# Attention and two gated layers on one core: six units of 384 tokens in place of eight of 288

## The chip, the cores and the metric

The kernel runs on one core of one Trainium2 chip. The metric is the device time of one execution in microseconds, from all inputs in HBM to the last output row in HBM. Lower is better.

## What is computed

Three parts follow one another. The inputs are 4 sequences of 576 tokens, 8 heads of 64.

```python
def _attn_ref(q, k, v, w1, b1, w2):            # 4 x 8 x 576 x 64
    scores = scale * np.matmul(q, k.transpose(0, 1, 3, 2))
    rel = (pos[:, None] - pos[None, :]).astype(np.float32)
    x = (np.log1p(np.abs(rel)) / np.log1p(np.maximum(pos[:, None], 1.0)))[..., None]
    bias = np.maximum(x @ w1 + b1, 0.0) @ w2    # one 576 x 576 table for each head
    scores = scores + bias.transpose(2, 0, 1)[None]
    attn = np.exp(scores - np.max(scores, axis=-1, keepdims=True))
    attn = attn / (np.sum(attn, axis=-1, keepdims=True) + 1e-09)
    return np.matmul(attn, v)
def _moe_ref(x, w_in, w_out):                   # 2304 x 512, inner 2048
    h = x @ w_in
    return (h - np.tanh(h)) @ w_out
def _moe2_ref(x, w_gate, w_val, w_out):         # inner 1536
    g = x @ w_gate
    return (g * (1.0 / (1.0 + np.exp(-g))) * (x @ w_val)) @ w_out
```

## The kernel before, in words

All products are made from operands that are split in a high part (type fp32r) and a low part (the rest). A product of weights and activations is three matmuls (high by high, high by low, low by high). For the scores the high and the low part of q lie in the two halves of the partitions, so a score tile is two matmuls for each half of the keys.

**Stages.** (1) The bias tables are computed in 36 rounds and written to HBM (`bias_scratch`). (2) Attention alone for the first 8 heads. (3) The first layer of unit u beside the attention of unit u+1. (4) The first layer of the last unit alone, while the weights of the second layer are loaded and split. (5) The second layer on 6 blocks of 384 tokens; its result leaves from PSUM through ScalarE.

**Units.** A unit is 288 tokens, one half of a sequence. There are 8 (`UNITS`), with 8 heads each. The queries of a head are cut into three tiles of 96 rows (`QT`, `NQ`). The keys are 576 in five chunks of 128; the fifth starts at key 448, so its first 64 keys are there twice, and v has zeros for them.

**One tile of a head.** TensorE makes the scores (`scores`, L1077, 4 matmuls of 288 columns). VectorE adds the bias and takes the row maximum (`score`, L878). ScalarE takes the exponential and the row sum (`exp_tile`, L646). VectorE inverts the sum (`inverse`, L885 and L888). GpSimd multiplies the rows by it (`norm`, L546). TensorE transposes the tile in five pieces into PSUM (`transposed`, L1090). ScalarE copies the high part (`pt_high`, L654), and VectorE subtracts it for the low part (`pt_low`, L893). When the three tiles of a head are ready, TensorE multiplies them by v (`output`, L1100, ten matmuls of 288 columns, five for the high part and five for the low part); ScalarE copies one half of the result to other partitions (`o_part`, L670), and VectorE adds the other half (`x_out`, L906). GpSimd splits k (L529, L531) and v (L538, L540).

**One chunk of the first layer.** There are 16 chunks of 128 hidden values. `hidden_pieces` (L1124) is 4 pieces of 3 matmuls into `ps_h`; then `tanh` (ScalarE, L659), `gated` (VectorE, L899), `g_high` (ScalarE, L664), `split_g` (GpSimd, L551), and `model_pieces` (L1143), again 4 pieces of 3 matmuls, into `ps_y`.

**The order of the work** is written out by hand. A slot is one call of a function `slot` on each engine; every engine runs its own list in order. In stage 3 a slot holds the attention of one head and two chunks of the layer. On TensorE it is: transposes of tile 0 of the head before, scores of tile 0, 4 pieces; the same for tile 1, 4 pieces; for tile 2, 3 pieces; then `output`, then the pieces that are left. In stage 2 a slot has no pieces, and TensorE makes `output` of the head before the last ahead of the transposes. There `output` goes to `ps_y`, and tiles 0, 1 and 2 are transposed into three different banks; in stage 3 all three tiles and `output` share the bank `ps_pt`.

At the end of a unit VectorE copies `x_stage` to `x_hi` (`x_high`, L915) and subtracts for `x_lo` (`x_low`, L920). The result of a unit goes from `ps_y` through ScalarE (`y_out`, L676) to `y_stage` and by DMA to HBM (`store_y`). The 28 weight tiles of the first layer that are not split in stage 1 are split in the slots of the first unit, four to a slot: four copies on ScalarE (`w1_high`, L613), three subtractions on VectorE (`w1_low`, L839) and one on GpSimd (L556).

Units 1 to 5 of stage 3 and pairs of blocks of stage 5 are loops of the program (`Fori`, L329 and L341); the first unit, the last two and the last two blocks are written out. All DMAs are issued by SyncE in one order: for each head v, k, q, and three bias tiles (`load_head`, L402).

## Time and profile before

| | us |
|---|---|
| median of 3 runs | 1258.95 (1256.47 to 1260.03) |
| the profiled execution | 1256.5 |
| its span, first to last instruction | 1254.4 |
| TensorE busy | 1194.2 (95%) |
| VectorE, ScalarE, GpSimd busy | 637.9, 595.3, 573.3 |
| granted TensorE clock, mean | 0.992 |

The profiled execution lies 2.1 us above its own span and 2.5 us below the median of the runs. "Busy" is the time in which at least one instruction of the engine ran; matmuls overlap, so the mean duration of one matmul is longer than its share of the busy time, and the pace is better read from the start of one group to the start of the next.

### The profile page before, as it was taken

To read this page: it belongs to the slowest core of one execution; us is meant where nothing else is said; L and a number is where in the kernel's file an instruction comes from. 1 tells how busy PE (TensorE), PEld (TensorE's weight loads), DVE (VectorE), ACT (ScalarE), POOL (GpSimd) and SP (SyncE) were. 2 spreads that over 40 slices of the span, in tenths; PEclk is the share of its full clock that TensorE was granted. 3 is DMA by queue.
4 is the path that set the end of the run, shared out by engine and by line. 5 is a ranking of instruction groups with operands and counts; after the bars stand their busy time and mean duration, and the time that the engine had idled before them with its cause. 6 is when DMAs were issued, how large, how long until landed. Compare 5 with 4: busy or idle time off the path is not lost.

```text
span 1254.4 us, 25061 instructions
## 1 busy us (share of the span) xinstructions
PE 1194.2 (95%) x8400; PEld 1127.0 (90%) x8400; DVE 637.9 (51%) x1575; ACT 595.3 (47%) x1301; POOL 573.3 (46%) x664
## 2 busy tenths in 40 slices
PE   5767799999999999999999999999999999999999
PEld 2346699999999999999999999999999999999998
DVE  8967888666666666666666644521211212112111
ACT  6966687655655656555656545521212222122212
POOL 2047699666666766776666644211111111111111
PEclk9989899999999999999999999999999999999999
DMA  5888354444444443444444434300100000000000
GB/s 165 242 257 244 107 182 122 129 123 123 141 122 122 140 120 109 135 120 128 121 119 137 123 125 152 120 26 1 40 11 25 25 25 25 0 26 1 26 1 26
DMA packets 69153, 125.01 MB, mean 100 GB/s; under 512 B 8544, under 2 KB 32096, under 8 KB 69088
## 3 DMA queue, kind: packets, MB, share of 16 engines
q1 hardware_dynamic: 69088, 124.16, 33.4%
q8 instruction: 39, 0.64, 0.2%
q14 instruction: 26, 0.21, 0.1%
HBM read 104.07 MB, written 20.05 MB: 99 GB/s over the span
## 4 chain that ended last, share of the span: by engine, by line
PE 84%; DVE 5%; issue 3%; POOL 3%; ACT 3%; DMA 1%; SPq 1%; POOLq 0%; DVEq 0%
PE ps_h L1124 14%; PE ps_y L1143 14%; PE ps_s L1215 12%; PE ps_y L1226 12%; PE ps_s L1077 7%; PE ps_h L1215 6%; PE ps_pt L1215 6%; PE ps_pt L1090 6%; PE ps_pt L1100 5%; DVE feat L847 3%; POOL fr L551 1%; POOL prob L546 1%; DVE prob L878 1%; ACT wbuf L654 1%; DVE wbuf L893 1%
## 5 line engine op out<-in xcount | busy, mean ns | idle before, releaser
L588 POOL TENSOR_TENSOR fr<-x_stage,fr 128x384 fp32r<-128x384 f32 x72 | 72.9, 1012 | 380.1 <-ACT fr L777 380.1
L546 POOL TENSOR_SCALAR prob<-prob,rowinv 96x576 f32<-96x576 f32 x192 | 149.6, 784 | 197.6 <-DVE rowinv L888 196.9
L1143 PE MATMUL ps_y<-fr,wbuf 128*128 128x288 f32 x1536 | 225.4, 295 | 1.1 <-POOL fr L551 0.4
L1124 PE MATMUL ps_h<-fr,wbuf 128*128 128x288 f32 x1440 | 219.9, 296 | 0.7 <-DVE fr L920 0.7
L1143 PEld LDWEIGHTS ps_y<-fr,wbuf 128*128 128x128 f32 x1536 | 210.4, 188 | 2.9 <-POOL fr L551 2.8
L1124 PEld LDWEIGHTS ps_h<-fr,wbuf 128*128 128x128 f32 x1440 | 201.1, 189 | 1.7 <-issue 1.0
L893 DVE TENSOR_TENSOR wbuf<-ps_pt,wbuf 128x480 fp32r<-128x480 f32 x176 | 115.6, 657 | 151.2 <-ACT wbuf L654 150.6
L654 ACT ACTIVATE wbuf<-ps_pt 128x480 fp32r<-128x480 f32 x176 | 100.5, 571 | 185.2 <-PE ps_pt L1090 185.0
L1226 PE MATMUL ps_y<-wbuf,fr 128*128 128x512 f32 x648 | 162.1, 395 | 0.0
L646 ACT ACTIVATE prob<-prob,negmax 96x576 f32<-96x576 f32 x192 | 147.8, 770 | 10.2 <-DVE negmax L878 10.1
L551 POOL TENSOR_TENSOR fr<-g_b,fr 128x288 fp32r<-128x288 f32 x128 | 112.2, 876 | 79.2 <-ACT fr L664 79.1
L1226 PEld LDWEIGHTS ps_y<-wbuf,fr 128*128 128x128 f32 x648 | 120.8, 188 | 22.8
L878 DVE CUSTOM_DVE_ANT_0 prob<-ps_s,biasb 96x576 f32<-96x576 f32 x179 | 133.2, 744 | 2.8 <-PE ps_s L1077 2.2
L1077 PE MATMUL ps_s<-wbuf,fr 128*96 128x288 f32 x672 | 126.2, 310 | 2.5 <-DVE negmax L878 2.5
L1023 DVE TENSOR_TENSOR x_stage<-ps_h,x_stage 128x384 f32<-128x384 f32 x36 | 20.1, 557 | 180.8 <-ACT x_stage L774 180.8
L1090 PE MATMUL ps_pt<-ident,prob 96*128 96x96 f32 x880 | 102.9, 247 | 7.4 <-POOL prob L546 5.4
L1023 DVE TENSOR_TENSOR x_stage<-ps_s,x_stage 128x384 f32<-128x384 f32 x36 | 20.1, 557 | 160.8 <-ACT x_stage L774 160.8
L1090 PEld LDWEIGHTS ps_pt<-ident,prob 96*128 96x128 f32 x880 | 90.8, 141 | 11.0 <-POOL prob L546 6.7
L1077 PEld LDWEIGHTS ps_s<-wbuf,fr 128*96 128x96 f32 x672 | 86.4, 164 | 4.3 <-DVE negmax L878 4.3
L531 POOL TENSOR_TENSOR wbuf<-k_raw,wbuf 128x576 fp32r<-128x576 f32 x59 | 86.8, 1471 | 4.9
L774 ACT ACTIVATE x_stage<-ps_h 128x384 f32<-128x384 f32 x36 | 17.7, 491 | 141.7 <-PE ps_pt L1215 141.7
L1100 PE MATMUL ps_pt<-wbuf,fr 128*128 128x288 f32 x560 | 83.2, 295 | 0.0
(111 smaller groups left out, 1832.0 us busy)
## 6 DMA issues: line engine op xcount, KB each, us to landing
biasb<-bias_scratch SPq DMA_DIRECT2D x192, 216.0 KB, 3.9
k_raw<-k_t SPq DMA_DIRECT2D x59, 288.0 KB, 2.8
bias_scratch<-w_raw SPq DMA_DIRECT2D x72, 144.0 KB, 2.8
v_raw<-v_p SPq DMA_DIRECT2D x64, 160.0 KB, 3.4
q_raw<-q_t SPq DMA_DIRECT2D x59, 144.0 KB, 2.6
w_raw<-w_chunks SPq DMA_DIRECT2D x16, 512.0 KB, 6.1
prob<-w_chunks SPq DMA_DIRECT2D x8, 768.0 KB, 4.2
y_scratch<-y_stage SPq DMA_DIRECT2D x8, 576.0 KB, 4.5
```

Source lines behind the costliest of these rows:

```text
L546: eng.tensor_scalar(prob[0:QT, par, t, :], prob[0:QT, par, t, :], rowinv[0:QT, par, t:t + 1], 1.0, ALU.mult, ALU.mult).then_inc(p_norm, 1)
L551: eng.tensor_tensor(g_lo[i], g_b[:, i, :], g_hi[i].bitcast(F32), ALU.subtract).then_inc(p_glo, 1)
L646: eng.activation(prob[0:QT, par, t, :], prob[0:QT, par, t, :], ACT.Exp, scale=-1.0, bias=negmax[0:QT, par, t:t + 1], accum_out=rowsum[0:QT ...
L878: eng.tensor_tensor_reduce(out=pairs(prob[0:QT, par, t, :]), in0=score_bank(par, t, moe)[0:QT, :, 0:T1], in1=pairs(biasb[0:QT, par, t, :]) ...
L893: eng.tensor_tensor(pt_lo[:, :, cols], by_chunk(bank), pt_hi[:, :, cols].bitcast(F32), ALU.subtract)\
L1077: mm = eng.matmul(bank[0:QT, a, 0:T1], q[:, t * QT:(t + 1) * QT], k[:, a * T1:(a + 1) * T1], start=i == 0, stop=i == 1)
L1090: mm = eng.transpose(bank[:, c * QT:(c + 1) * QT], prob[0:QT, par, t, KEY0[c]:KEY0[c] + P], ident[0:QT, 0:QT])
L1100: mm = eng.matmul(bank[:, 0:T1], vv[:, c, :, :].rearrange("p a d -> p (a d)"), pt[:, c, :], start=i == 0 and c == 0, stop=i == 1 and c == ...
L1124: mm = eng.matmul(hidden_bank(u, c)[:, 0:T1], w[:, cols], x[:, d, :], start=d == 0 and i == 0, stop=d == KC - 1 and i == 2)
L1143: mm = eng.matmul(ps_y[:, d, 0:T1], w[:, cols], g[c % 2], start=c == 0 and i == 0, stop=c == C1 - 1 and i == 2)
L1215: mm = eng.matmul(bank, w[:, cols], y[:, d, :], start=d == 0 and i == 0, stop=d == KC - 1 and i == 2)
L1226: mm = eng.matmul(ps_y[:, t, :], a[c % 2][:, t * P:(t + 1) * P], w, start=c == 0 and i == 0, stop=c == C2 - 1 and i == 2)
```

## The change

**Units.** There are six units of 384 tokens (`TOK`, `PARTS`). Units 0 to 3 are the first 384 tokens of each sequence: 8 heads each, of three tiles of 128 rows. Units 4 and 5 are the last 192 tokens of two sequences: 16 heads each, of two tiles of 96 rows. Heads stay 64 in all; tiles are 160 (were 192). In stage 3 a slot of units 0, 1 and 2 holds a head of 384 tokens and two chunks of the layer; a slot of units 3 and 4 holds a head of 192 tokens and one chunk.

**Keys.** A tile of 128 rows is transposed in four pieces of 128 keys. The last 64 keys of its three tiles are transposed together behind the third tile (`transposed_end`, three transposes into `ps_pt`); ScalarE copies the high part into one half of the partitions of `pt_end`, VectorE puts the low part into the other half, v has its last 64 keys in both halves, and one matmul serves for both parts. `output` of such a head is nine matmuls of 384 columns; of a head of 192 tokens it is ten of 192.

**Order.** In stage 3 ScalarE now does `exp_tile` and `tanh` ahead of the next tile's `pt_high`, and VectorE `inverse` and `gated` ahead of the next `pt_low`. `x_high` goes to ScalarE for three of its four chunks.

**Storage.** `prob` is a ring of 6 tiles, `biasb` a ring of 4. `x_stage` and `y_stage` are one buffer: `y_out` of unit u-1 waits for `x_low` of unit u, and the first `o_part` of unit u+1, in the same slot, waits for the store of y, which is now two or more DMAs (its first chunk by itself). `o_part` writes into `x_stage` itself. A bias tile of 128 rows is two DMAs, q of a long head two, v three.

**Loads.** Eight of the 16 weight chunks of the first layer are loaded in stage 1 (were six), the others from head 9 on. The first four bias tiles are loaded behind round 27 (were three).

**Loops.** The loops over units and blocks are written out.

```diff
-UNITS = 2 * B
-HEADS = UNITS * H
+TOK = 384
+PARTS = B * S // TOK
+def list_heads():
+    heads, tiles = [], 0
+    for u in range(PARTS):
+        pieces = [(u, 0, TOK // P, P)] if u < B else [(2 * (u - B) + i, TOK, (S - TOK) // QT, QT) for i in range(2)]
+        for h in range(H):
+            for i, (seq, row0, nt, rows) in enumerate(pieces):
+                heads.append(Head(len(heads), u, h, seq, row0, i * nt * rows, nt, rows, tiles))
+                tiles += nt
+    return heads, tiles
...
         def slots(slot, edge):
+            for u in range(PARTS):
+                attended = HEADS[FIRST_OF[u + 1]:FIRST_OF[u + 2]] if u + 1 < PARTS else [None] * H
+                per = C1 // len(attended)
+                for j, v in enumerate(attended):
+                    after = HEADS[v.n + 1:v.n + 3] if v is not None else []
+                    q, p = (after + [None, None])[:2]
+                    slot(q, v, p, [(u, j * per + i) for i in range(per)])
...
+            def transposed_end(hd, moe):
+                eng.wait_ge(v_pt, rounds(hd, hd.nt if moe else 1))
+                for t in range(hd.nt):
+                    mm = eng.transpose(ps_pt[:, tile_cols(hd, t)], prob[:, (hd.tile0 + t) % PR, S - P:S], ident[:, :])
+                mm.then_inc(e_pt, 1)
+            def output(hd, moe):
+                eng.wait_ge(v_pt, all_rounds(hd))
...
+                for part in range(2):
+                    for c in range(chunks_of(hd)):
+                        mm = eng.matmul(bank, vv[:, c, :, :]..., pt_of(hd, part)[:, c, :], ...)
+                if ended(hd):
+                    mm = eng.matmul(bank, vv[:, FULL, :, :]..., pt_end, start=False, stop=True)
```

The slot on TensorE:

```diff
+            def slot(q, v, p, moe):
+                pieces = []
...
+                gaps = ([4, 0, 2] if moe[0] == (0, 0) else [4, 4, 2]) if len(moe) == 2 else [4, 2]
+                for t, gap in enumerate(gaps):
+                    if v is not None and t < v.nt:
+                        transposed(v, t, moe)
+                    if q is not None and t < q.nt:
+                        scores(q, t, moe)
+                    layer_work(gap)
+                if v is not None:
+                    if ended(v):
+                        transposed_end(v, moe)
+                        layer_work(3)
+                    output(v, moe)
                 layer_work(len(pieces))
```

The slot on ScalarE in stage 3 (`when[i]` is the tile number behind which chunk i's tanh stands):

```diff
+                for t in range(end + 1):
+                    if t < v.nt:
+                        pt_high(v, t, moe)
+                    for k in (tiles[-1:], tiles[1:2], [])[t]:
+                        w1_high(k)
+                    if t == 1 and ends_unit:
+                        y_out(moe[0][0] - 1)
+                    for i, (u, c) in enumerate(moe):
+                        if when[i] == t - 1:
+                            g_high(u, c)
+                    if t == end:
+                        if p is not None:
+                            q_high(p, moe)
+                        if ended(v):
+                            pt_high_end(v)
+                        if one:
+                            o_part(v, moe)
+                    if q is not None and t < q.nt:
+                        exp_tile(q, t)
+                    for k in (tiles[0:1], tiles[2:3], [])[t]:
+                        w1_high(k)
+                    for i, (u, c) in enumerate(moe):
+                        if when[i] == t:
+                            tanh(u, c)
```

The slot on VectorE in stage 3, and the two waits that the shared buffer brings to ScalarE:

```diff
+                for t in range(end + 1):
+                    if t < v.nt:
+                        pt_low(v, t, moe)
+                    if q is not None and t < q.nt:
+                        score(q, t, moe)
...
+                    if t == end:
+                        if ended(v):
+                            pt_low_end(v)
+                        if p is not None:
+                            q_low(p, moe)
+                        if one:
+                            x_out(v, moe)
+                    if q is not None and t < q.nt:
+                        inverse(q, t)
+                    for k in (tiles[0:1], tiles[1:2], [])[t]:
+                        w1_low(k)
+                    for i, (u, c) in enumerate(moe):
+                        if when[i] == t:
+                            gated(u, c)
...
+            def o_part(hd, moe):
+                if hd.unit > 1:
+                    eng.wait_ge(d_y_first if hd.h < 2 else d_y_rest, Y_SUM[hd.unit - 1])
             def y_out(u):
+                eng.wait_ge(v_xlo, 2 * min(u + 2, PARTS))
```

## Rows read from the trace of the kernel before

**Rows 1.** The page's first part: busy time, share of the span, instructions

```profile
PE 1194.2 (95%) x8400; PEld 1127.0 (90%) x8400; DVE 637.9 (51%) x1575; ACT 595.3 (47%) x1301; POOL 573.3 (46%) x664
```

**Rows 2.** Busy time by stage: stretch, length, five engines (x), PEclk, DMA share, GB/s

```profile
0.00:76.00 76.00, 50.70 (x609) 25.49 (x609) 67.05 (x139) 62.38 (x91) 7.75 (x15) 1.00 0.72 214
76.00:143.60 67.60, 43.88 (x296) 38.24 (x294) 51.24 (x143) 38.36 (x90) 48.34 (x60) 0.87 0.75 219
143.60:740.00 596.40, 590.04 (x4720) 584.91 (x4720) 395.20 (x1095) 368.26 (x883) 422.21 (x502) 1.00 0.44 125
740.00:797.70 57.70, 55.93 (x406) 53.97 (x405) 26.76 (x33) 30.20 (x51) 22.11 (x17) 1.00 0.51 175
797.70:1254.40 456.70, 453.61 (x2377) 424.38 (x2375) 97.66 (x167) 96.10 (x190) 72.87 (x72) 1.00 0.06 21
```

**Rows 3.** Timeline of TensorE in one slot of stage 3: start, us, engine, line

```profile
429.05 1.49 PE L1100 MATMUL ps_pt<-wbuf,fr 128*128 128x288 f32 x10
...
430.77 1.74 PE L1143 MATMUL ps_y<-fr,wbuf 128*128 128x288 f32 x12
432.36 0.58 PE L1090 MATMUL ps_pt<-ident,prob 96*128 96x96 f32 x5
432.71 0.75 PE L1077 MATMUL ps_s<-wbuf,fr 128*96 128x288 f32 x4
433.30 1.75 PE L1124 MATMUL ps_h<-fr,wbuf 128*128 128x288 f32 x12
...
437.43 0.58 PE L1090 MATMUL ps_pt<-ident,prob 96*128 96x96 f32 x5
...
439.57 1.49 PE L1100 MATMUL ps_pt<-wbuf,fr 128*128 128x288 f32 x10
```

**Rows 4.** Chain that ended last, stage 5: start, us, what

```profile
810.40 2.11 PE ps_pt L1215 x12
812.51 2.10 PE ps_y L1226 x9
```

**Rows 5.** Timeline of ScalarE and VectorE, end of the same slot

```profile
438.05 0.57 ACT L654 ACTIVATE wbuf<-ps_pt 128x480 fp32r<-128x480 f32 x1 [0.93 <-PE ps_pt L1090]
...
438.65 0.66 DVE L893 TENSOR_TENSOR wbuf<-ps_pt,wbuf 128x480 fp32r<-128x480 f32 x1 [0.60 <-ACT wbuf L654]
```

**Rows 6.** Groups by line: xcount | busy us, mean ns of one | idle before

```profile
L613 ACT ACTIVATE wbuf<-w_raw 128x512 fp32r<-128x512 f32 x32 | 18.5, 622 | 0.0
L839 DVE TENSOR_TENSOR wbuf<-w_raw,wbuf 128x512 fp32r<-128x512 f32 x25 | 20.1, 804 | 0.0
```

**Rows 7.** Timeline of TensorE at the first slot of units 1 and 3

```profile
228.49 0.60 PE L1090 MATMUL ps_pt<-ident,prob 96*128 96x96 f32 x5 [0.92 <-POOL prob L546]
...
400.16 0.60 PE L1090 MATMUL ps_pt<-ident,prob 96*128 96x96 f32 x5 [0.92 <-POOL prob L546]
```

**Rows 8.** Timeline of VectorE and GpSimd in stage 4

```profile
784.39 1.75 DVE L928 TENSOR_TENSOR wbuf<-prob,wbuf 128x1536 fp32r<-128x1536 f32 x1
785.03 1.77 POOL L551 TENSOR_TENSOR fr<-g_b,fr 128x288 fp32r<-128x288 f32 x1 [2.75 <-ACT fr L664]
```

**Rows 9.** Groups of GpSimd by line

```profile
L546 POOL TENSOR_SCALAR prob<-prob,rowinv 96x576 f32<-96x576 f32 x192 | 149.6, 784 | 197.6 <-DVE rowinv L888 196.9
L551 POOL TENSOR_TENSOR fr<-g_b,fr 128x288 fp32r<-128x288 f32 x128 | 112.2, 876 | 79.2 <-ACT fr L664 79.1
```

**Rows 10.** Timeline of VectorE and TensorE in stage 2

```profile
79.84 0.75 DVE L878 CUSTOM_DVE_ANT_0 prob<-ps_y,biasb 96x576 f32<-96x576 f32 x1 [3.62 <-DMA biasb<-bias_scratch]
...
129.84 0.66 DVE L893 TENSOR_TENSOR wbuf<-ps_y,wbuf 128x480 fp32r<-128x480 f32 x1 [0.56 <-ACT wbuf L654]
130.56 1.58 PE L1100 MATMUL ps_y<-wbuf,fr 128*128 128x288 f32 x10 [1.29 <-DVE wbuf L893]
...
137.74 2.77 PE L1100 MATMUL ps_y<-wbuf,fr 128*128 128x288 f32 x10 [3.83 <-DVE wbuf L893]
```

**Rows 11.** Timeline of SyncE's queue in a slot of stage 3

```profile
433.96 1.36 SPq L399 DMA_DIRECT2D biasb<-bias_scratch  x3
```

More of the change, by code:

```diff
@@ L347, in attention_layers_kernel, with steps @@
+        def steps(step):
+            for v in range(V2):
+                step(v, v % 2, v == V2 - 1)
         SPLIT_AT = 4
@@ L581, in _ @@
             eng.sem_inc(p_alo, 1)
-            slots(eng, slot, None)
-            with eng.Fori(0, V2) as v:
+            slots(slot, None)
+            for v in range(V2):
                 for c in range(C2):
@@ L969, in slot @@
-                if qk:
-                    inverse(n, par, 0)
-                for k in tiles[1:2]:
-                    w1_low(k)
-                if pv:
-                    pt_low(n - 1, 2, banks[2])
-                if qk:
-                    score(n, par, 2, moe)
-                    inverse(n, par, 1)
-                if prep:
-                    q_low(n + 1, 1 - par, moe)
-                if pv and not last:
-                    x_out(n - 1, 1 - par, o_bank, x_chunk)
-                w2_lows(w2_splits[0])
@@ L986, in slot @@
+                if not one:
+                    x_out(v, moe)
                 for k in tiles[2:3]:
                     w1_low(k)
-                w2_lows(w2_splits[1])
-                if pv and last:
-                    x_high(moe[0] + 1, 0)
-                    x_out(n - 1, 1 - par, o_bank, x_chunk)
-                    x_low(moe[0] + 1, 0)
-                    x_high(moe[0] + 1, 1)
-                    x_low(moe[0] + 1, 1)
-                if qk and last:
-                    inverse(n, par, 2)
+                if late(moe):
+                    x_low(moe[0][0] + 1, 0)
@@ L1197, in _ @@
             eng.sem_inc(e_out, 2)
-            slots(eng, slot, edge)
-            for piece in model_pieces(UNITS - 1, C1 - 1):
+            slots(slot, edge)
+            for piece in model_pieces(PARTS - 1, C1 - 1):
                 piece()
```

1012 lines of the change are left out of this document (522 added, 490 removed).

## The prediction

> **What bounds the kernel now.** I read the page's busy line first: TensorE is busy for 95% of the span, no other engine for more than 51% [rows 1]. By stage [rows 2]: bias tables 76 us, attention alone 67.6, layer beside attention 596.4, the last unit alone 57.7, second layer 456.7. TensorE is busy for 99% of the third and the last, but for only 65% of the second, where its clock also drops (mean 0.87). So three fifths of the time is a question of TensorE's instructions, and stage 2 is one of waits between engines.
>
> The pace is read from starts. One slot of stage 3 takes 10.52 us from `output` to `output`, without a wait [rows 3]. In it five transposes take 0.36 (0.072 each), four scores 0.585, and twelve layer matmuls of 288 columns 1.60 (0.133 each). `output` takes 1.33 (ten at the same 0.133). In stage 5 twelve matmuls of 384 columns take 2.11 (0.1758 each) and nine of 512 take 2.10 (0.2335) [rows 4]. A line through the three is 6 to 7 ns per matmul plus 0.44 ns per column: the cost follows the columns, and little is fixed. The skill page "TensorE: Matmul & The Clock Gate" (Back-to-back issue gap) gives N/2.4 + 2.5 ns, so a smaller fixed part; by it the removal of 768 matmuls would bring 2 us where my line brings 5. My sum uses the rows.
>
> **TensorE's work from slot 9 to the second layer.** Before: 56 slots of 10.52 are 589.1, and 32 groups of 1.60 for the last unit 51.2; sum 640.3. The stretch is 654.1 (143.6 to 797.7 [rows 2]), and the transposes and scores of its first slot lie ahead of it, 1.9 at the low clock (twice 0.36 + 0.585). So some 15.7 us of 656.0 are stalls.
> After:
> - Layer: 6 units x 32 groups x 2.11 = 405.1 (was 409.6).
> - Long head: scores 3 x 0.585 = 1.76; fifteen transposes of 128 columns. Bounds for one are 0.072 (the row, if the load sets it) and 0.096 (in proportion to columns); I take 0.080, nearer to the row of the same 128-column load: 1.20. Nine matmuls of 384 are 1.58. Sum 4.54, for 24 heads 108.9 (bounds 106 to 115).
> - Short head: 2 x (0.36 + 0.585) and ten matmuls of 192 columns, between 0.072 and 0.133, 0.091 by the line: 2.80, for 32 heads 89.6 (84 to 103).
> Sum 603.6, which is 36.7 less. A long slot becomes 12.98, a short one 7.02.
>
> **Stalls of that stretch, after.**
> - Every slot: what `output` waits for. Now the last tile's transposes start at 437.43, its copy at 438.05, and the subtraction ends at 439.31, 1.88 later; `output` comes 2.14 behind the transposes [rows 3, 5]. That leaves 0.26. After, a short slot has 0.36 + 0.585 + six matmuls (1.055) = 2.00 there. The long slot has 2.04 ahead of the packed transposes, which reuse the bank, against about 1.97 (longer transposes and copies). The work queued ahead of the copy also changes: an exponential and tanh now come first. Walking both slots through, each on its own list, I find the copies just in time. I take 0.1 a slot, 5 us; bounds 0 and 0.6 a slot (34 us).
> - First unit: three weight copies of 0.62 on ScalarE and two subtractions of 0.80 on VectorE [rows 6] now stand between tile 0's exponential and tile 2's subtraction. My walk gives a stall of 1.2 a slot, for seven slots 8.4; bounds 0 and 1.9 a slot.
> - Unit ends: now a unit's first transposes wait 0.92 for `norm` [rows 7]. After, the shared x/y buffer puts `o_part` of the first head behind `y_out` and a store. In the long slots (13 us) this is hidden. In a short slot `ps_y` is complete about 3.1 in, the first copy waits for `x_low`, and its DMA lands some 3 us later. I take 3 us at each of two such ends, 0.6 at two long ones, 1.7 at the last: 9 (bounds 4 and 15).
> - Last unit: `split_g` takes 1.77 where VectorE runs a weight subtraction of 1.75 [rows 8] and 0.88 in the mean [rows 9]. With 2.11 a group the round trip of about 3.9 fits under two groups (4.22); before, about 3.45 stood against 3.2. So 1 us is left of it. Start of the stage, clock low: 3.
> Sum 26.4, 10.7 more than now.
>
> **Stage 2.** Tiles stay 27, since 128 rows cost the lanes what 96 do. A slot takes 7.18 (130.56 to 137.74), and TensorE waits 1.29 ahead of its first `output`, for the last `pt_low`: the subtraction starts at 129.84, `output` 0.72 later [rows 10]. After, the inverse (0.37) and the packed subtraction (about 0.5) stand between, +0.82; `output` itself +0.25, wider copies +0.27. That is +1.34 a slot for seven slots, 9.4, and 1 more at the edges. Against it, the first tile of head 1 no longer waits 3.62 for its bias [rows 10]: it is loaded with head 0's. Its second tile is still late, so I count 2.5. The weight loads that leave this stage give 1.2. Net +6.7 (bounds 0 and +19, the upper one if the clock drops).
>
> **At nothing.** Stages 1 and 5 do the same work; their TensorE and VectorE shares cover the moved buffers, and a copy or store late by less than a group of 2.1 us would not show. SyncE issues 12 DMAs in a long slot (6 in 10.5 us now); at 0.45 each [rows 11] that is 5.4 of 13 us, and in a short slot five make 2.3 of 7. Its bias ring of four tiles is loaded as each is used, some 10 us ahead of need. **Loops:** the first slot after the first unit, which is written out, waits 0.92, and so does one inside the loop [rows 7]; a pass of the loop costs TensorE nothing, so writing it out saves nothing. The skill page "Runtime: NRT & Kernel Launch" (Instruction fetch mechanics) says that a taken branch can stall the fetch and prefers unrolled code; by it there would be a gain here. The trace shows no such stall, and the sum has none.
>
> **Sum.** -36.7 + 10.7 + 6.7 = -19.3. From the profiled execution, 1256.5, that is 1237.2. It was 2.5 below the median of its runs, so a median would be 1239.7; I say 1239.
>
> **Rivals.**
> - *Round trip exposed (slower), 0.14.* Each slot's `output` or packed transposes wait for the last copy and subtraction, because ScalarE and VectorE have the exponential, tanh and `gated` ahead of them. For: the spare falls from 0.26 to about 0.1, with more queued ahead. Against: both engines are idle a third of stage 3 [rows 2]. It decides from 0.35 us a slot over 56 slots, which eats the gain. At 0.6 instead of 0.1: +28, 1267.
> - *GpSimd bounds the short slots, 0.12.* It has 422.2 us in 56 slots [rows 2], 7.54 each; less one `norm` (0.78) and one `split_g` (0.88), with the other a third wider (+0.29) [rows 9], that is 6.2 of 7.02. If its instructions stretch as in [rows 8], a short slot becomes 7.5 or more: +16, 1255. The skill page "SBUF — State Buffer" (SBUF: two separate sides) says that GpSimd and a VectorE instruction with two SBUF inputs exclude each other for a whole instruction; by this rule, with which 1.77 beside 1.75 agrees, `q_low` and `x_low` would block it.
> - *Half clock in stage 2, 0.10.* At the low clock `output` took 2.77 [rows 10], against 1.33. TensorE's share of a slot falls from 58% to some 53%, so drops may be more frequent. +1.6 for seven slots: 1250.
> - *Stalls as before, 0.15.* First unit and unit ends are covered as now, the transposes cost 0.072: -13, 1226.
> - *Fixed cost is nil* (the wide matmul saves nothing): the layer stays 409.6, +4.5. This lies in the range, since the gain is mostly attention's.
> The forecast has 0.49.
>
> **How the numbers follow.** A measurement of this kernel tells some 0.3%, 3.8 us, from no change: the same is 1255.2 to 1262.7. Faster: forecast 0.49, stalls as before 0.15, clock 0.09, half of GpSimd 0.06: 0.79. Same: the rest of GpSimd and 0.02 of the others: 0.08. Slower 0.13. The range leaves out most of the slower rival and the lowest gains: 1224 to 1260.
>
> **What would show it.** Right: starts of layer groups 2.11 apart, long slots 12.9 to 13.2, short ones 7.0 to 7.3, first-unit slots near 14.2, stage 2 slots near 8.5, second layer at 779 (was 797.7). Wrong: `output` or the packed transposes waiting for `pt_low` by over 0.3 in each slot; scores waiting for `split_k` (L531) in short slots; a stretch of stage 2 at half clock; a stage 5 other than 457 long.

## The result, and the profile after

The changed kernel takes 1265.7 us, median of four runs (1264.4 to 1266.0); the kernel before took 1258.5 beside it. The ratio is 1.0056, 95% interval 1.0039 to 1.0074: **slower by 0.6%, where 1.6% faster was forecast**. Its profiled execution took 1264.4 us with a span of 1262.6.

First the busy line of the page, then busy time by stage: bias tables, attention alone, layer beside attention, last unit, second layer. It answers to [rows 1, 2].

```profile
PE 1185.2 (94%) x7312; PEld 1094.9 (87%) x7312; DVE 635.8 (50%) x1401; ACT 576.3 (46%) x1171; POOL 540.2 (43%) x600
```

```profile
core 0: us, PE busy (x) PEld busy (x) DVE busy (x) ACT busy (x) POOL busy (x), PEclk, DMA share, GB/s
76.00:155.50 79.50, 52.38 (x283) 46.49 (x282) 55.06 (x148) 45.38 (x98) 48.35 (x59) 0.86 0.61 176
155.50:739.00 583.50, 563.92 (x3662) 533.05 (x3661) 388.30 (x917) 338.64 (x744) 386.48 (x438) 1.00 0.43 128
739.00:808.20 69.20, 67.21 (x384) 66.60 (x385) 27.29 (x32) 33.15 (x50) 24.21 (x16) 1.00 0.39 135
808.20:1262.60 454.40, 451.25 (x2378) 422.62 (x2376) 97.52 (x167) 96.23 (x189) 73.04 (x72) 1.00 0.06 22
```

Stage 2 grew from 67.6 to 79.5 us. Stages 3 and 4 together took 652.7 against 654.1: the 26 us that they were to give are not there. Stage 5 gave 2.3. The busy shares hide it: TensorE shows 97% of stage 3 busy, but a group that waits in its middle counts as busy, so the pace has to be read from starts again. From one first `output` matmul to the next:

| slots | before | forecast | after |
|---|---|---|---|
| stage 2, seven | 7.2 (one 7.6, one 8.4) | 8.52 | 8.6 (three), 9.05 (two), 9.6 (two) |
| first unit (long heads) | 10.52 | 14.28 | 14.40 |
| long heads, units 1 and 2 | 10.52 | 13.08 | 13.43 |
| short heads | 10.52 | 7.12 | 7.71 |
| unit end, two slots, long / short | 22.6 | 26.8 / 17.2 | 28.3 / 18.2 and 18.4 |

Against the forecast the short slots owe 0.59 x 32 = 18.9 us, the long ones 0.35 x 16 = 5.6, stage 2 5.2; less the 2.3 of stage 5 that makes 27.4, and the miss is 1264.4 - 1237.2 = 27.2. So the question is the short slot. These are the rows of one (timeline, all engines; the last column is idle time before and its releaser):

```profile
542.30 0.60 PE L1208 MATMUL ps_pt<-ident,prob 96*128 96x96 f32 x5 [0.21 <-DVE xy_stage L1028]
542.94 0.57 ACT L738 ACTIVATE wbuf<-ps_pt 128x480 fp32r<-128x480 f32 x1 [0.62 <-PE ps_pt L1208]
543.55 0.66 DVE L1009 TENSOR_TENSOR wbuf<-ps_pt,wbuf 128x480 fp32r<-128x480 f32 x1 [0.85 <-ACT wbuf L738]
544.12 0.74 DVE L993 CUSTOM_DVE_ANT_0 prob<-ps_s,biasb 96x576 f32<-96x576 f32 x1
544.91 0.78 ACT L731 ACTIVATE prob<-prob,negmax 96x576 f32<-96x576 f32 x1 [1.39 <-DVE negmax L993]
545.81 0.15 DVE L1002 TENSOR_SCALAR rowsum<-rowsum 96x1 f32<-96x1 f32 x1 [0.94 <-ACT prob L731]
546.37 0.75 POOL L617 TENSOR_SCALAR prob<-prob,rowinv 96x576 f32<-96x576 f32 x1 [1.32 <-DVE rowinv L1004]
547.08 0.67 POOL L599 TENSOR_SCALAR wbuf<-raw 128x576 fp32r<-128x576 f32 x1
547.36 1.36 PE L1225 MATMUL ps_pt<-wbuf,fr 128*128 128x192 f32 x10
547.83 1.43 POOL L601 TENSOR_TENSOR fr<-raw,wbuf 128x576 fp32r<-128x576 f32 x1
548.01 1.47 DVE L967 SCALAR_TENSOR_TENSOR fr<-raw,fr 64x192 fp32r<-64x192 f32 x1
548.56 1.23 PE L1271 MATMUL ps_y<-fr,wbuf 128*128 128x384 f32 x6
548.82 0.32 ACT L764 ACTIVATE xy_stage<-ps_pt 64x192 f32<-64x192 f32 x1 [1.26 <-PE ps_pt L1225]
549.51 0.36 DVE L1028 TENSOR_TENSOR xy_stage<-ps_pt,xy_stage 64x192 f32<-64x192 f32 x1
550.01 0.60 PE L1208 MATMUL ps_pt<-ident,prob 96*128 96x96 f32 x5 [0.22 <-DVE xy_stage L1028]
```

Two things stand here. **The output matmuls** take 548.56 - 547.36 = 1.20 for ten, 0.120 each and not 0.091. And **the first transposes wait**: L1271's six matmuls would be done at 549.6, and the next slot's L1208 starts at 550.01. It uses `ps_pt`, which `x_out` (L1028) must have emptied. `o_part` (L764) is ready at 549.14, but `x_out` stands behind `q_low` (L967), which took 1.47 us for 64x192, and that ended as GpSimd's `split_k` (L601) did.

Follow the rows from the top and each link starts as the one before it ends (only `q_low` starts earlier and ends with `split_k`), over four engines, until the transposes come again: copy, subtraction, score, exponential, inverse, norm, `split_k`, `q_low`, `x_out`. It is a closed loop, 7.71 us long. TensorE's own work in a slot is 7.3. That was only a reading so far; the runs below test it.

The long slot waits at the same place, 0.2, as I read it for another reason: `o_part` is queued behind `g_high` (L755), whose gate comes late. No run moved `g_high` by itself.

```profile
308.55 0.53 ACT L755 ACTIVATE fr<-g_b 128x384 fp32r<-128x384 f32 x1 [1.01 <-DVE g_b L1020]
308.57 1.72 PE L1271 MATMUL ps_y<-fr,wbuf 128*128 128x384 f32 x9
309.10 0.49 ACT L764 ACTIVATE xy_stage<-ps_pt 64x384 f32<-64x384 f32 x1
309.62 0.55 DVE L1028 TENSOR_TENSOR xy_stage<-ps_pt,xy_stage 64x384 f32<-64x384 f32 x1 [1.11 <-ACT xy_stage L764]
310.32 0.63 PE L1208 MATMUL ps_pt<-ident,prob 128*128 128x128 f32 x4
```

### The profile page after: what moved, and what is told of

The parts are those of the page before. It is cut to its first block, busy times and chain, and to the rows that moved or that the text cites. A ratio compares the mean times of both kernels' runs of the same rounds, so it can differ in the third digit from the quotient of the medians.

```text
span 1262.6 us, 20294 instructions
## 1 busy us (share of the span) xinstructions
PE 1185.2 (94%) x7312; PEld 1094.9 (87%) x7312; DVE 635.8 (50%) x1401; ACT 576.3 (46%) x1171; POOL 540.2 (43%) x600
## 4 chain that ended last, share of the span: by engine, by line
PE 64%; DVE 18%; issue 8%; ACT 8%; SPq 1%; DMA 1%; DVEq 0%; POOL 0%; ACTq 0%
PE ps_s L1341 12%; PE ps_y L1352 12%; PE ps_y L1271 9%; PE ps_h L1252 8%; PE ps_h L1341 6%; PE ps_pt L1341 6%; DVE prob L993 5%; PE ps_pt L1208 4%; DVE fr L967 3%; DVE feat L960 3%; PE ps_pt L1225 2%; ACT wbuf L738 2%; DVE wbuf L1009 2%; PE ps_s L1192 2%; DVE g_b L1020 2%
## 5 line engine op out<-in xcount | busy, mean ns | idle before, releaser
L1271 PE MATMUL ps_y<-fr,wbuf 128*128 128x384 f32 x1152 | 226.2, 337 | 2.0 <-ACT xy_stage L777 1.3
L617 POOL TENSOR_SCALAR prob<-prob,rowinv 128x576 f32<-128x576 f32 (+1 forms) x160 | 127.8, 799 | 207.6 <-DVE rowinv L1004 190.9
L1252 PE MATMUL ps_h<-fr,wbuf 128*128 128x384 f32 x1056 | 206.8, 340 | 1.8 <-DVE g_b L1020 1.8
L1271 PEld LDWEIGHTS ps_y<-fr,wbuf 128*128 128x128 f32 x1152 | 198.8, 188 | 2.6 <-POOL fr L622 2.6
L731 ACT ACTIVATE prob<-prob,negmax 128x576 f32<-128x576 f32 (+1 forms) x160 | 124.1, 776 | 103.8 <-DVE negmax L993 102.6
L622 POOL TENSOR_TENSOR fr<-g_b,fr 128x384 fp32r<-128x384 f32 x96 | 108.4, 1129 | 110.9 <-ACT fr L755 110.9
L1009 DVE TENSOR_TENSOR wbuf<-ps_pt,wbuf 128x512 fp32r<-128x512 f32 (+1 forms) x144 | 97.0, 674 | 58.6 <-ACT wbuf L738 57.5
L993 DVE CUSTOM_DVE_ANT_0 prob<-ps_s,biasb 128x576 f32<-128x576 f32 (+1 forms) x147 | 109.8, 747 | 6.9 <-issue 4.0
L738 ACT ACTIVATE wbuf<-ps_pt 128x512 fp32r<-128x512 f32 (+1 forms) x144 | 83.3, 579 | 51.4 <-PE ps_pt L1208 50.2
L1208 PE MATMUL ps_pt<-ident,prob 128*128 128x128 f32 (+1 forms) x640 | 88.8, 266 | 12.1 <-DVE xy_stage L1028 10.7
L1208 PEld LDWEIGHTS ps_pt<-ident,prob 128*128 128x128 f32 (+1 forms) x640 | 70.8, 143 | 31.4 <-issue 26.4
L601 POOL TENSOR_TENSOR fr<-raw,wbuf 128x576 fp32r<-128x576 f32 x59 | 85.0, 1441 | 4.9
```

Source lines behind the costliest of these rows:

```text
L617: eng.tensor_scalar(row, row, rowinv[0:hd.rows, tile % PR:tile % PR + 1], 1.0, ALU.mult, ALU.mult).then_inc(p_norm, 1)
L622: eng.tensor_tensor(g_lo[c % 2], g_b[:, c % 2, :], g_hi[c % 2].bitcast(F32), ALU.subtract)\
L731: eng.activation(row, row, ACT.Exp, scale=-1.0, bias=negmax[0:hd.rows, col], accum_out=rowsum[0:hd.rows, col]).then_inc(a_exp, 1)
L738: eng.activation(pt_of(hd, 0)[:, :, tile_cols(hd, t)], by_chunk(pt_bank(t, moe), hd), ACT.Copy)\
L993: eng.tensor_tensor_reduce(out=pairs(prob[rows, i, :]), in0=score_bank(tile, moe)[rows, :, 0:T1], in1=pairs(biasb[rows, tile % BR, :]), sc ...
L1009: eng.tensor_tensor(lo, by_chunk(pt_bank(t, moe), hd), hi.bitcast(F32), ALU.subtract).then_inc(v_pt, 1)
```

## Experiments

All but the last two start from the changed kernel (1265.7). Slot times are differences of starts in each run's own profile.

### Is x_out late, and by whom? e1_one_input

In the short heads' `q_low`, one operand instead of two; the low half of their q is left out of the result.

```diff
+                if not ended(hd):
+                    eng.tensor_scalar(q, src[64:P, 0:width(hd)], float(D) ** -0.5, 1.0, ALU.mult, ALU.mult)
+                    return
                 eng.scalar_tensor_tensor(q, src[64:P, 0:width(hd)], ...)
```

> The low half of q of the 32 short heads is left out: q_low (L967) becomes one tensor_scalar with a single SBUF input, in the same place of VectorE's list. Theory A (q_low, which reads two SBUF operands, is held by GpSimd's split_k low, and x_out, and with it the next slot's first transposes, stand behind it): q_low falls from 1.47 us to under 0.5, x_out starts as o_part ends, the wait of 0.22 on xy_stage before the transposes goes, and a short slot falls from 7.71 to about 7.35; 32 of them make -11 to -12, 1254 us. Rival B (the slot's length is set by something else, such as o_part's place on ScalarE or TensorE's own work): q_low may get shorter, the slots stay within 0.1 of 7.71, 1265 us. Rival C (GpSimd holds any VectorE instruction on SBUF, one input or two): q_low stays at 1.4.

Measured 1263.4 us; `q_low` takes 1.37 us, a short slot 7.61.

```profile
543.33 1.43 POOL L601 TENSOR_TENSOR fr<-raw,wbuf 128x576 fp32r<-128x576 f32 x1
543.50 1.37 DVE L968 TENSOR_SCALAR fr<-raw 64x192 fp32r<-64x192 f32 x1
544.90 0.36 DVE L1032 TENSOR_TENSOR xy_stage<-ps_pt,xy_stage 64x192 f32<-64x192 f32 x1
```

Rival C: with one SBUF input VectorE is held as well, and finishes 0.11 us after GpSimd's instruction ends (544.87 and 544.76). My condition of two inputs was wrong for this form. The slot fell by the same 0.10 that `q_low` lost, so `q_low` does lie on what sets the slot. The Trainium skill, "SBUF — State Buffer" (SBUF: two separate sides), has one more case: the lock that the two engines share is taken also by a VectorE instruction in a two-port mode. The row agrees in so far as this one was held; that it ran in such a mode, no row shows.

### What makes the output matmuls long? e2_narrow_v

Short heads' output with 64 columns of weights; the low half of their v is left out.

```diff
-  mm = eng.matmul(bank, vv[:, c, :, :]..., pt_of(hd, part)[:, c, :], ...)
+  mm = eng.matmul(bank[0:64, :], vv[:, c, 0, :], pt_of(hd, part)[:, c, :], ...)
```

> The low half of v of the short heads is left out: their ten output matmuls have 64 columns of weights instead of 128, the same 192 moving columns. Theory A (the weight load sets the 0.120 us that a matmul of 192 columns takes with 128 columns of weights): each falls to about 0.091, the ten to 0.9 from 1.20, but the short slot stays at 7.7, because x_out behind the held q_low still ends at the same time. Rival B (a fixed cost of a change of weights or of the bank, whatever their width): 0.120 stays. If A holds and the slot falls by 0.3 too, x_out is not what ends it.

```profile
540.87 1.10 PE L1225 MATMUL ps_pt<-wbuf,fr 128*64 128x192 f32 x10
541.80 1.25 PE L1273 MATMUL ps_y<-fr,wbuf 128*128 128x384 f32 x6
543.51 0.60 PE L1208 MATMUL ps_pt<-ident,prob 96*128 96x96 f32 x5 [0.46 <-DVE xy_stage L1028]
```

One run, 1264.8 us. As theory A had it: ten take 0.93, and the slot stays at 7.71, the wait ahead of the transposes grows from 0.22 to 0.46 instead. The moving columns are the same 192, so the difference of 0.027 comes from the weight side. Not all of the 0.120 does: in e5 and e6 below, where the last subtraction ends 0.12 and 0.11 ahead of `output` and not 0.05, ten take 1.14 and 1.13. "TensorE: Matmul & The Clock Gate" in the Trainium skill (Back-to-back issue gap) says that the spacing is set by both instructions of a pair; the two rows agree, and my line through three wide matmuls knew only one of them. (The formula that the prediction quotes from there is given for a matmul alone, not for such a stream.)

### Undoing the wait at TensorE: e3_scores_first

```diff
                 for t, gap in enumerate(gaps):
+                    if t == 0 and q is not None:
+                        scores(q, 0, moe)
                     if v is not None and t < v.nt:
                         transposed(v, t, moe)
-                    if q is not None and t < q.nt:
+                    if t > 0 and q is not None and t < q.nt:
                         scores(q, t, moe)
```

> Only TensorE's order changes: in every slot beside the layer, the scores of the next head's first tile (0.585 us) go ahead of the first transposes, which wait for x_out since both use one bank. Theory A (each slot loses 0.35 (short) or 0.2 (long) to that wait, because x_out is late): short slots 7.71 to about 7.35, long ones 13.44 to about 13.25, unit ends shorter by up to 0.6; together -14 to -17, 1250 us. Rival B (the wait is only one of several that end together: GpSimd's or ScalarE's round takes over): under 5 us gained, and another wait of 0.2 to 0.3 in the short slots, on split_k, q_low or norm.

A miss on both sides: 1276.4 us, short slots 7.84, long 13.57, first unit 14.82. The wait before the transposes is gone and another of 0.34 stands before `output`:

```profile
547.67 1.36 PE L1225 MATMUL ps_pt<-wbuf,fr 128*128 128x192 f32 x10 [0.34 <-DVE wbuf L1009]
550.47 0.58 PE L1208 MATMUL ps_pt<-ident,prob 96*128 96x96 f32 x5
555.51 1.36 PE L1225 MATMUL ps_pt<-wbuf,fr 128*128 128x192 f32 x10 [0.33 <-DVE wbuf L1009]
```

The first loop no longer binds: `x_out` (549.82 to 550.18) is done 0.29 ahead of the transposes. A second one does. From the first transposes over copy, subtraction, score, exponential, tanh, the second tile's copy and its subtraction (L1009) to `output` it is 5.04 us, as before; then TensorE itself needs 1.20 for `output`, 1.06 for six layer matmuls and now 0.54 for the scores, until it comes to the next transposes. That is 7.84. In the changed kernel this way was just covered: from the transposes to `output` TensorE's own work, scores among it, filled 5.06. The scores, put ahead of the transposes, no longer run beside the other engines' 5.04 but are added to it.

### The order on VectorE: e5_both_orders and e6_vector_order

e6 changes VectorE's order alone; e5 is e3 and e6 together.

```diff
                 for t in range(end + 1):
+                    if t == 0 and q is not None:
+                        score(q, 0, moe)
                     if t < v.nt:
                         pt_low(v, t, moe)
-                    if q is not None and t < q.nt:
+                    if t > 0 and q is not None and t < q.nt:
                         score(q, t, moe)
```

> TensorE's order as in e3_scores_first (scores of the next head's first tile ahead of the first transposes), and besides VectorE takes that score ahead of the first tile's subtraction. Theory A (two chains of equal length end a short slot: from the first transposes over copy, subtraction, score, exponential, tanh, copy, subtraction to the output matmuls, 5.04 us from start to start in after, e1 and e3 alike, and from output over o_part and x_out to the next transposes, 2.65; e3 only moved the wait from the second to the first): with score ahead the first chain shortens by 0.5 or more, both are then covered by TensorE's own work of 5.05 + 2.25, and a short slot takes 7.3 to 7.4 (was 7.71), a long one 13.2 to 13.3 (13.44): -14 to -17, 1250 us. Rival B (GpSimd's round, split_k behind norm, ends the slot): short slots stay at 7.6 or more, with a wait on split_k low or q_low ahead of the scores.

> Only VectorE's order of e5 (score ahead of the first tile's subtraction), TensorE's as in the changed kernel. Theory A (in the changed kernel the chain that binds TensorE is output, o_part, x_out, transposes; the other is just covered): short slots stay at 7.6 to 7.71, since TensorE's own work from the first transposes to output (5.05) does not shrink: 1262 to 1266 us. Rival B (the order of score and subtraction alone is what is wrong): short slots fall to 7.4, 1254 us.

e5 took 1244.9 us (ratio to before 0.9885, 0.9869 to 0.9902), e6 1249.4 (0.9924, 0.9906 to 0.9943). Short slots are 7.27 and 7.31, long ones 13.22 and 13.33. e5's slots came out as expected; its total is 5 us under what I had named, since the first unit's slots fell too (14.40 to 13.84). In a short slot of e5 TensorE has no wait:

```profile
546.71 1.30 PE L1227 MATMUL ps_pt<-wbuf,fr 128*128 128x192 f32 x10
547.85 1.23 PE L1273 MATMUL ps_y<-fr,wbuf 128*128 128x384 f32 x6
```

But e6 refutes the theory with which I expected it: of the two chains that I saw, score is in only one, and yet it moved the other. e6's rows show how:

```profile
540.67 0.74 POOL L617 TENSOR_SCALAR prob<-prob,rowinv 96x576 f32<-96x576 f32 x1 [0.53 <-DVE rowinv L1004]
541.43 0.67 POOL L599 TENSOR_SCALAR wbuf<-raw 128x576 fp32r<-128x576 f32 x1
542.19 1.42 POOL L601 TENSOR_TENSOR fr<-raw,wbuf 128x576 fp32r<-128x576 f32 x1
542.72 1.11 DVE L967 SCALAR_TENSOR_TENSOR fr<-raw,fr 64x192 fp32r<-64x192 f32 x1
543.89 0.36 DVE L1028 TENSOR_TENSOR xy_stage<-ps_pt,xy_stage 64x192 f32<-64x192 f32 x1
```

`output` starts at 542.14 here, so the second instruction of `split_k` begins 0.05 behind it instead of 0.47, `q_low` is held for 1.11 instead of 1.47, and `x_out` starts as `o_part` ends. With the score a subtraction (0.66) earlier, exponential, inverse and norm are earlier, and with them `split_k`. It is one loop through four engines that binds here, not two chains. Shortened, it falls under TensorE's own 7.3; and in e3's loop the first tile's copy and subtraction then no longer stand ahead of the score, so that e5 can have both orders without a wait.

### Cutting the loop elsewhere: e9_split_first

```diff
+                if p is not None and q.nt == 2:
+                    split_k(p, moe)
                 for t in range(last):
                     if t == last - 1:
-                        if p is not None:
+                        if p is not None and q.nt > 2:
                             split_k(p, moe)
```

> Only GpSimd's order, in the slots of short heads: split_k goes ahead of both norms instead of between them. Theory A, revised by e6 (a short slot of the changed kernel is one closed loop of waits: first transposes, copy, subtraction, score, exponential, inverse, norm, split_k, the held q_low, x_out, first transposes; the links sum to 7.71 and TensorE needs 7.31): with split_k off the loop it is cut, q_low is released earlier, and a short slot falls to 7.3 to 7.4, 32 of them -10 to -13: 1253 to 1256 us, nearly what e6 gave by another cut. Rival B (e6 gained because the exponential and tanh come earlier for pt_high, and GpSimd has no part in it): slots stay at 7.6 to 7.7, 1264 us.

1260.7 us (1.0016, 1.0007 to 1.0026), short slots 7.45; a smaller gain than expected (7.3 to 7.4, 1253 to 1256 us). GpSimd alone was reordered, and the slot fell by 0.26. The loop is shown, from three sides: e1 took 0.10 out of a link and the slot lost 0.10, e6 and e9 took a link out. `split_k` now waits for the second scores (`[1.34 <-PE ps_s L1194]`), and `q_low` is still held, but no longer late: in a slot of e9 `o_part` ends at 580.28 and `x_out` starts at 580.31. What is left is the way `output` (578.50), `o_part`, `x_out`, next transposes (580.88), 2.38 us against the 2.24 of TensorE's own work there. So of the 0.40 in the changed kernel, 0.26 belonged to the held `q_low` and 0.14 to this other way. In e6 it is 2.26, with `output` itself 0.07 shorter.

### Stage 2: e4_end_early and e7_stage2_order

The chain of a stage-2 slot, in the changed kernel:

```profile
130.35 0.69 DVE L1009 TENSOR_TENSOR wbuf<-ps_y,wbuf 128x512 fp32r<-128x512 f32 x1 [0.56 <-ACT wbuf L738]
130.96 0.14 DVE L1002 TENSOR_SCALAR rowsum<-rowsum 128x1 f32<-128x1 f32 x1
131.33 0.56 DVE L1013 TENSOR_TENSOR wbuf<-ps_pt,wbuf 64x384 fp32r<-64x384 f32 x1
131.95 1.33 PE L1225 MATMUL ps_y<-wbuf,fr 128*128 128x384 f32 x6 [2.17 <-DVE wbuf L1013]
```

That is the forecast's addition, inverse and packed subtraction behind the last `pt_low`, at its forecast price. e4 puts the packed copy and subtraction (L743, L1013) ahead of the third tile's; e7 also takes the first exponential ahead of `o_part` and the second score ahead of `x_out`.

```diff
                         if v is not None:
                             pt_high(v, t, moe)
+                            if t == 1:
+                                pt_high_end(v)
...
                         inverse(q, t)
+                        if v is not None and t == 1:
+                            pt_low_end(v)
```

And e7 besides, with the like on VectorE (`score` of tile 1 ahead of `x_out`):

```diff
-                    if q.n >= 2:
-                        o_part(HEADS[q.n - 2], moe)
                     for t in range(q.nt):
                         exp_tile(q, t)
+                        if t == 0 and q.n >= 2:
+                            o_part(HEADS[q.n - 2], moe)
```

> Stage 2 alone: the packed keys' copy goes ahead of tile 2's exponential on ScalarE, their subtraction ahead of tile 2's subtraction on VectorE, where that engine is idle 0.56 us. Theory A (the packed end costs a stage-2 slot what stands between tile 2's subtraction and the first output matmul, the inverse of 0.37 and the subtraction of 0.56): seven slots fall by 0.9 each, 8.62 to about 7.7, so -6.5; with fewer drops of the clock up to -10; 1256 to 1259 us. Rival B (the wider slot comes from the 128-row tiles and wider copies, or from the output matmuls at the low clock): under 2 us, slots stay over 8.3.

> Stage 2 only: e4_end_early, and besides the exponential of tile 0 goes ahead of o_part on ScalarE, and the score of tile 1 ahead of x_out on VectorE; both now stand idle (2.9 and 1.5 us) behind the output matmuls. Theory A (after e4 a slot of 7.93 at full clock is a chain output, o_part, exponential of tile 0, copy, subtraction): a slot loses 0.8 to 1.3 more, to about 7.0, and with TensorE busier fewer slots meet the low clock: 7 to 12 us under e4's 1259, 1247 to 1252. Rival B (another chain, over norm of the last tile and its transposes, is as long): under 3 us gained, slots at 7.6 or more.

e4: 1259.1 us (0.9998, 0.9987 to 1.0010). Slots at full clock 7.93, 0.7 less, but others still 9.1. e7: 1253.4 us (0.9955, 0.9939 to 0.9971), five slots of 7.26 in a row. e7's gain over e4 is 5.7, less than the 7 expected at least. In e4's profile four of the seven slots still met the low clock, with waits of 0.9 to 1.5 ahead of `output`. What the low clock costs is seen in the changed kernel's own rows, the same `output` in two slots:

```profile
86.45 1.66 PE L1225 MATMUL ps_y<-wbuf,fr 128*128 128x384 f32 x8 [1.19 <-DVE wbuf L1013]
95.06 2.52 PE L1225 MATMUL ps_y<-wbuf,fr 128*128 128x384 f32 x8 [2.16 <-DVE wbuf L1013]
```

The second started after 2.16 us of waiting, at a granted clock of 0.57 in 95 to 99 us (mostly the 1.2 GHz level, then); the one at 113.72, after the same wait, took 1.68. Four of the seven slots are longer than 8.62; that adds 2.8 us of the 11.2 by which the seven grew (63.2 against 52.0, first to last `output`). How many slots meet it differs between executions: the last `output` of this stage came at 149.6 in the profile of the changed kernel and at 151.2 to 153.8 in those of e1, e3, e5, e6, e8, e9 and e11, whose stage 2 is the same.

### The first unit: e8_weights_later

```diff
-                    for k in (tiles[0:1], tiles[2:3], [])[t]:
+                    for k in tiles[0:1] if t == 0 else []:
                         w1_high(k)
...
                             tanh(u, c)
+                for k in tiles[2:3]:
+                    w1_high(k)
```

(and on VectorE `w1_low` of `tiles[1]` behind the last `gated`)

> First unit only: of the four weight tiles split in a slot, the third one's copy goes on ScalarE from ahead of the last tile's copy to behind the last tanh, the second one's subtraction on VectorE from ahead of the last tile's subtraction to behind the last gated. Theory A (as in the forecast, the weight splits queued ahead of tile 2's subtraction make the 0.8 us wait ahead of the packed transposes): first-unit slots fall from 14.40 to 13.5 to 13.7, seven of them -5 to -6, 1260 us. Rival B (GpSimd's norm, 1.25 beside VectorE's weight subtraction, or the first transposes' wait for x_out make it): slots stay over 14.0.

1264.7 us; slots 14.14 instead of 14.40. The wait ahead of the packed transposes fell as meant, but only 0.26 of it reached the slot:

```profile
206.80 0.55 PE L1215 MATMUL ps_pt<-ident,prob 128*128 128x128 f32 x3 [0.79 <-DVE wbuf L1009]
```

```profile
209.80 0.55 PE L1219 MATMUL ps_pt<-ident,prob 128*128 128x128 f32 x3 [0.27 <-DVE wbuf L1011]
```

Neither theory holds whole. With e5's orders instead these slots are 13.84, and 13.60 in e10, which has both.

### Unit ends: e11_store_apart

The stores of two units send other bytes, so the shared x/y buffer is free at once; their result is left out.

```diff
+                    if u in (2, 3):
+                        eng.dma_start(y_d[:, chunks, u * S:u * S + TOK], w2_chunks[0, :, 0:n * TOK]...)
...
+                if hd.unit >= 4:
+                    eng.wait_ge(a_y, (hd.unit - 1) * KC + CR_Y)
```

> The stores of the layer's results of units 3 and 4 send rows of a weight array instead (same sizes, same queue), so that the first heads' o_part at the two ends with short slots need not wait until the store has read the shared x/y buffer; what is stored for these two units is left out. Theory A (the shared buffer makes the second slot of such an end 9.64 to 9.72 long, by o_part's wait of 1.6 for the store): these slots fall to 8.0 to 8.3, the two ends together -2.5 to -3.5. Rival B (y_out itself, four copies behind x_low, holds o_part as long): over 9.

One run, 1263.9 us. The second slots fall from 9.64 and 9.72 to 8.51 twice, so the buffer costs 1.1 to 1.2 at each, less than expected, and another 0.8 of the slot is something else. In the changed kernel, then in e11:

```profile
494.03 0.33 ACT L764 ACTIVATE xy_stage<-ps_pt 64x192 f32<-64x192 f32 x1 [1.57 <-DMA y_scratch<-xy_stage]
494.88 0.60 PE L1208 MATMUL ps_pt<-ident,prob 96*128 96x96 f32 x5 [1.01 <-DVE xy_stage L1028]
```

```profile
494.77 0.33 ACT L770 ACTIVATE xy_stage<-ps_pt 64x192 f32<-64x192 f32 x1 [0.44 <-PE ps_pt L1231]
496.34 0.60 PE L1214 MATMUL ps_pt<-ident,prob 96*128 96x96 f32 x5 [0.57 <-DVE xy_stage L1034]
```

### All orders together: e10_combined

e5, e7 and e8 in one kernel, with the changed kernel's tiles and buffers.

> All orders together: e5_both_orders, e7_stage2_order and e8_weights_later; the computation, the tiles and the buffers are those of the changed kernel. Theory A (the parts are independent, each in its own stage): 1265.7 - 20.8 (e5) - 12.3 (e7) - 1.0 (e8) = 1231.6, so 1229 to 1235 us, 2% under the kernel before. Rival B (the start of stage 3 meets the low clock or a late load once stage 2 is shorter): 1236 to 1242.

**1230.4 us, ratio 0.9777 (0.9763 to 0.9790): 2.2% under the kernel before and 35 us under the changed one.** The parts add (1231.6 by the sum). Its stages:

```profile
76.00:143.00 67.00, 48.45 (x282) 42.62 (x280) 54.34 (x146) 45.58 (x97) 50.55 (x60) 0.88 0.69 194
143.00:705.10 562.10, 554.37 (x3665) 538.49 (x3665) 384.84 (x920) 345.11 (x745) 385.25 (x439) 1.00 0.47 135
705.10:774.20 69.10, 67.11 (x384) 66.50 (x385) 27.26 (x32) 33.13 (x50) 24.21 (x16) 1.00 0.39 135
774.20:1228.60 454.40, 451.26 (x2378) 422.64 (x2376) 97.40 (x167) 96.19 (x189) 73.04 (x72) 1.00 0.06 22
```

Stages 3 and 4 are 631.2, against 654.1 before: the 23 us that the six units give once the waits are out. That the total lies under the forecast's 1239 does not confirm the forecast: TensorE's work is some 14 us more than it had, and stage 2 has an order that it knew nothing of.

### Would the kernel before have gained as much? e12_before_orders and e13_before_stage2

e12 puts the same four orders (score, scores, first exponential, second score) into the kernel before; e13 only the two of stage 2.

```diff
-                    if pv and not first:
-                        o_part(n - 2, par, o_bank)
                     for t in range(NQ):
                         exp_tile(n, par, t)
+                        if t == 0 and pv and not first:
+                            o_part(n - 2, par, o_bank)
```

> The kernel before (eight units of 288), with those orders of e10 that it has a place for: in stage 2 the exponential of tile 0 ahead of o_part and the score of tile 1 ahead of x_out, beside the layer the score ahead of the first subtraction and the scores ahead of the first transposes. It asks whether e10's 28 us come from the orders alone or need the change. Theory A (before has no wait in a stage-3 slot of 10.52, so the orders bring only stage 2, 7 slots of 7.2 to about 6.3): 1250 to 1254 us, and e10, 1230, owes some 20 us to the six units. Rival B (the orders would have brought as much without the change): 1240 or less, stage-3 slots under 10.4.

> The kernel before with only the two stage-2 orders of e12: exponential of tile 0 ahead of o_part, score of tile 1 ahead of x_out. e12 mixed them with two stage-3 orders that put the scores behind GpSimd's split_k (slots 10.87 instead of 10.52). Theory A (the kernel before has nothing else to gain from orders, its stage-3 slots have no wait): stage-2 slots 6.8 instead of 7.2 at full clock, stage-3 slots 10.5, 1254 to 1258 us; then some 24 to 28 us of e10 need the six units, and the forecast's 36.7 us less TensorE work is real. Rival B (stage 2 alone brings the kernel before down by as much as e7 brought the changed one, 12): 1247 or less.

e12: 1276.9 us, a miss; its slots grew to 10.87. The scores now stand 0.36 us earlier in the list and meet `split_k`, which ends at 443.40:

```profile
441.97 1.43 POOL L531 TENSOR_TENSOR wbuf<-k_raw,wbuf 128x576 fp32r<-128x576 f32 x1
443.53 0.76 PE L1077 MATMUL ps_s<-wbuf,fr 128*96 128x288 f32 x4
```

e13: 1257.6 us, ratio 0.9994 (0.9983 to 1.0005), no difference. Stage-2 slots are 6.81 at full clock instead of 7.19, but two take 8.7, so the seven take 51.9 and not 52.0; stage 3 stays at 10.52. So e10's 28 us are not to be had from orders alone, as far as these two tried. The order that gave most in the changed kernel, VectorE's, was not tried here by itself; but a slot's matmuls and transposes by the prediction's prices, 3 x 0.945 + 1.33 + 4 x 1.60 = 10.57, already fill its 10.52.

## Why the prediction was wrong, by its own steps

- **TensorE's work, -36.7: right in kind, about 14 too much.** With the waits out (e5) a short slot is 7.27 and a long one 13.22, where I had 7.02 and 12.98. Short: the output matmuls take 1.14, not 0.91, +0.23 (0.114 each; that the weight side has a part in it, e2 shows); the twelve layer matmuls behind the first transposes take 2.17, not 2.11, +0.06; the first scores 0.53, not 0.585. I had 0.133 as the upper bound of an output matmul and took the line instead of it. Long: fifteen transposes take 1.34, 0.088 to 0.097 each and not 0.080, +0.14, and the 48 layer matmuls 8.56, not 8.44, +0.12; scores and `output` cost what I had. Over all heads 32 x 0.25 + 24 x 0.24 = 13.8 are missing, so some 23 us are real, as e10's stages 3 and 4 have them.
- **"I find the copies just in time. I take 0.1 a slot": the step that failed.** The copies were in time, to within 0.05 (the subtraction ends at 547.31, `output` starts at 547.36). What was late is `x_out`, 0.40 in each short slot and 0.2 in each long one, 16 us. I walked through one slot from its first transposes to its `output` and never asked when the next slot's first transposes may start, though `ps_pt` serves both them and `output`. In the old slot fifteen layer matmuls of 288, 2.0 us, stood between the two [rows 3]; now there are six of 384, 1.04. I had put 5 us there, 11 too little. With the 13.8 above that is 24.8, and stages 3 and 4 missed by 24.6 (the smaller terms nearly cancel). Either error alone would have left the kernel faster than before: without the wait it is e5's 1244.9, and without the other, by this sum, some 1252.
- **First unit 14.28: right** (14.40), but more by luck than by its reason: over a long slot of 13.22 it is 1.2, of which moving two of the four weight tiles gave back 0.26 (e8) and the orders of e5 0.56.
- **Unit ends 3 at short ones, 0.6 at long ones:** 2.8 and 3.0, right; 1.4 at long ones, 0.8 too little each. Last unit 1.7 and 1: waits of 1.26 and 0.73, right.
- **Stage 2, +6.7: +11.9 in the profile.** A slot at full clock costs 8.62, forecast 8.52. What failed is the net: the low clock, which I had put at the edge of the range, takes 2.8 us, and the first `output` comes 0.7 later than before where I credited 2.5 for the bias load. The load comes for head 0's three tiles, but `score` of head 1's second tile starts at 81.02, after 4.0 us of waiting; the trace names no releaser, and the bias loads for it are issued from 77.40 on.
- **Nothing for stages 1 and 5 and for loops:** stage 1 as before; stage 5 gave 2.3. No wait went away there: TensorE's pace itself is a little quicker, nine matmuls of 512 take 2.08 in each block, where before they took 2.10 and 2.09 in turn, and twelve of 384 take 2.09 in the mean for 2.10. What sets this is open.
- **Rivals.** "GpSimd bounds the short slots" (0.12) had the right pair of engines, 16 us against the measured 12.8, but the wrong way round: VectorE's `q_low` waits for GpSimd's `split_k`, not `split_k` for `q_low`, and GpSimd itself is idle for more than a fifth of the slot (5.94 of 7.71 busy). "Round trip exposed" had the right size per slot (it named 0.35 as the point that decides) and the wrong place. "Half clock in stage 2" came true besides. I gave each its chance as if they excluded each other; three of them happened together, each with a part of its price.
- **A reading that was off:** the last and the third stage, where TensorE is 99% busy, are 84% of the span (596.4 and 456.7 of 1254.4 [rows 2]), not three fifths. Nothing in the sum rests on it.

## What to carry to other kernels

When slots become shorter, a work list in program order is not enough: follow the dependences from one operation around to the same operation of the next slot, through every engine and every shared bank, and compare the length of that loop with the bound engine's work. The old slot left such a loop 10.5 us, the new one 7.3. When a large saving of work does not show, look for the wait that comes back each slot at one place and for what is queued ahead of its releaser; here a single exchange of two VectorE instructions gave 16 us, and TensorE's own order, which looked like the direct remedy, cost 11, because it lengthened a second loop that had been just covered. Cutting one loop uncovers the next (7.71, then 7.45 in e9), so read the waits again after each step.

## What was unexpected of the hardware

- A VectorE instruction with a single SBUF input and an SBUF output (64x192) took 1.37 us beside a GpSimd instruction of 1.43 that had begun first (e1); with two inputs 1.47, and 0.51 where GpSimd's instruction ended 0.30 after it began (482.62 in the changed kernel).
- A matmul of 192 moving columns took 0.120 us with 128 columns of weights and 0.093 with 64 (e2), and 0.114 with 128 in e5; why e5's are shorter was not tried.
- In stage 2 of the changed kernel, with waits of 2.2 us ahead of `output`, four of seven slots met the low clock (six in e5, which has the same stage 2), in e7, with 1.46, one or two. But in e4, with at most 1.5, it was four, and in e13, with 1.28, two: the length of the wait alone does not say it, and none of these runs singles out a cause.
